# Attention, gated feed-forward and expert layer on one core: how the first unit is laid out, and who waits for the last scatters

## What is computed

```python
scores = scale * q @ k.T;  mask = (rel >= 0) & (rel < 64)      # rel = row - column
attn = softmax(where(mask, scores, -1e9)); a = attn @ v         # -> x [2304, 512]
xn = x / sqrt(mean(x*x) + 1e-6) * rms_g
y = (silu(xn @ w_gate) * (xn @ w_val)) @ w_out                  # 512 -> 1536 -> 512
e = argmax(y @ wg2);  p = softmax(y @ wg2)[e]
out[token] = p * (relu(y[token] @ w1[e]) @ w2[e])               # 512 -> 1024 -> 512
```

## Time and profile before

| | us |
|---|---|
| median of 3 runs | 842.87 (842.76 to 847.07) |
| the profiled execution | 843.32 |
| its span in the trace | 841.3 |

### The profile page before, as it was taken

The page is one execution under the profiler, slowest core; times in us unless marked ns, Lnnn a source line. Parts: engine busy times, 40 slices in busy tenths (PEclk is TensorE's granted clock), DMA queues, the critical chain, the costliest instruction groups (busy, mean ns, idle before and its releaser), DMA issues.

```text
span 841.3 us, 15268 instructions
## 1 busy us (share of the span) xinstructions
PE 818.7 (97%) x4803; PEld 732.0 (87%) x4804; DVE 483.2 (57%) x977; ACT 287.1 (34%) x664; POOL 214.3 (25%) x194
## 2 busy tenths in 40 slices
PE   6989999999999999999999999999999999999995
PEld 6877889999999999999999999998888888888884
DVE  5878822447764866676486667735315545564351
ACT  5767621321122121213212223334415435443440
POOL 5267799403000200300030000050831111111100
PEclk9999999999999999999999999999999999999998
DMA  6898880002002000200110012206354643654100
GB/s 207 252 316 260 300 328 39 1 1 76 1 0 76 1 1 3 76 1 1 34 42 1 1 39 101 100 28 239 118 180 150 217 156 138 248 192 178 53 19 20
DMA packets 38598, 88.22 MB, mean 105 GB/s; under 512 B 4030, under 2 KB 13246, under 8 KB 38016
## 3 DMA queue, kind: packets, MB, share of 16 engines
q1 hardware_dynamic: 33488, 72.89, 25.2%
q0 software_dynamic: 3360, 10.23, 3.4%
q10 hardware_dynamic: 1680, 4.21, 1.5%
HBM read 73.16 MB, written 14.94 MB: 105 GB/s over the span
## 4 chain that ended last, share of the span: by engine, by line
PE 92%; DMA 3%; ACT 1%; DVE 1%; issue 1%; POOL 1%; SPq 0%; POOLq 0%; ACTq 0%
PE ps L956 27%; PE ps L958 27%; PE ps L957 27%; PE ps L1094 2%; DMA kt<-kT 2%; PE ps L901 2%; PE ps L921 1%; PE ps L897 1%; PE ps L1015 1%; DMA xT_rows<-xo 1%; PE ps L909 1%; ACT pr L688 1%; PE ps L1131 0%; DVE nmax L1195 0%; PE ps L887 0%
## 5 line engine op out<-in xcount | busy, mean ns | idle before, releaser
L956 PE MATMUL ps<-xn_hi,GV_hi 128*128 128x384 f32 x576 | 195.6, 340 | 0.5 <-ACT pr L688 0.4
L958 PE MATMUL ps<-xn_hi,GV_lo 128*128 128x384 f32 x576 | 193.3, 336 | 0.0
L957 PE MATMUL ps<-xn_lo,GV_hi 128*128 128x384 f32 x576 | 193.0, 335 | 0.0
L956 PEld LDWEIGHTS ps<-xn_hi,GV_hi 128*128 128x128 f32 x576 | 108.2, 188 | 4.6 <-issue 0.6
L957 PEld LDWEIGHTS ps<-xn_lo,GV_hi 128*128 128x128 f32 x576 | 108.2, 188 | 3.3
L958 PEld LDWEIGHTS ps<-xn_hi,GV_lo 128*128 128x128 f32 x576 | 108.1, 188 | 0.0
L1291 DVE CUSTOM_DVE_ANT_0 ps<-ysb,wrb 128x512 f32<-128x512 f32 x120 | 91.9, 766 | 6.0 <-ACT ysb L750 1.0
L737 ACT ACTIVATE sig<-ps 128x384 f32<-128x384 f32 x72 | 35.4, 492 | 168.6 <-PE ps L958 168.5
L743 ACT ACTIVATE h_hi<-ps 128x384 fp32r<-128x384 f32 x72 | 35.4, 491 | 165.6 <-DVE ps L1261 165.6
L958 PE MATMUL ps<-Wo_hi,h_lo 128*128 128x512 f32 x216 | 85.5, 396 | 0.0
L957 PE MATMUL ps<-Wo_lo,h_hi 128*128 128x512 f32 x216 | 85.3, 395 | 0.0
(11 more groups left out here) (163 smaller groups left out, 1393.8 us busy)
## 6 DMA issues: line engine op xcount, KB each, us to landing
EW_raw<-w SPq DMA_DIRECT2D x32, 1024.0 KB, 5.7
vt<-vW SPq DMA_DIRECT2D x32, 192.0 KB, 5.1
qraw<-qT SPq DMA_DIRECT2D x16, 288.0 KB, 4.3
kt<-kT SPq DMA_DIRECT2D x16, 288.0 KB, 4.2
xT_rows<-xo SPq DMA_DIRECT2D x16, 288.0 KB, 3.6
y_rows<-ysb SPq DMA_DIRECT2D x6, 768.0 KB, 4.1
xraw<-xT_rows SPq DMA_DIRECT2D x5, 768.0 KB, 5.6
vt<-vW SPq DMA_DIRECT2D x16, 128.0 KB, 4.2
```

Source lines behind the costliest of these rows:

```text
L956: nc.tensor.matmul(out, a_hi, b_hi, start=start, stop=False)
L957: nc.tensor.matmul(out, a_hi, b_lo, start=False, stop=False)
L958: return nc.tensor.matmul(out, a_lo, b_hi, start=False, stop=stop)
```

## The change

At the head: q and k of unit 0 are loaded in two pieces each, the first job's columns (`FIRST`, three blocks, 192 columns) and the rest (`REST`, 384 columns). SP issues q's two pieces and k's rest before it raises its semaphores; ACT issues k's first piece before anything else, and `gvec` and `wr` only behind its first six jobs. `heads` is filled by VectorE with four fills; POOL cuts wider masks of 192 columns on all partitions in three selects, of which each half of the partitions takes its own 128 columns, and rounds the identity itself. VectorE copies the first mask, lays out the first piece of unit 0, copies the second mask, lays out the rest, and raises eight of its semaphores only then. TensorE multiplies job 0's scores before it adds the mask to them; in all other jobs the mask still comes first. POOL lays out unit 1 behind VectorE's lay-out, and waits for `gvec` and `wr` at unit 14.

In the middle: VectorE works out, for each of the four `osb` buffers, up to which count `o_out` must come (`landed_i`), and reads the four values into registers ahead of the slots.

At the tail: POOL waits for no landing. Its nested conditions are turned round, so that the last scatter stands in a condition of its own (`used == s + 1`) behind the block of the further levels. VectorE waits, behind its own last conditions, for the four counts and does a small instruction after each wait.

```diff
@@ build @@
-        mask_raw = r.take("mask_raw", 2, KEYS)
+        mask_raw = r.take("mask_raw", 2, WIN + KEYS)
@@ SP @@
+            sp.dma_start(qraw[0][:, FIRST], qT[0][:, FIRST]).then_inc(q_first, 16)
+            sp.dma_start(qraw[0][:, REST], qT[0][:, REST]).then_inc(q_in[0], 16)
+            sp.dma_start(kt[0][:, REST], kT[0][:, REST]).then_inc(k_in[0], 16)
             for s_ in (y_stored, *xT_out):
                 sp.sem_inc(s_, 16)
...
-            load_q(0, 0)
-            load_k(0, 0)
@@ POOL @@
-            for t, x in ((heads, 1.0), (ident, 0.0), (mask_raw, 0.0)):
-                g.memset(t[:], x).then_inc(blank, 1)
+            for t in (mask_raw, ident):
+                g.memset(t[:], 0.0).then_inc(blank, 1)
...
-            for half in halves:
...
+            select(mask_raw[:, 0, :], consts, compare_op=ALU.is_ge, fill=MASKED, base=0, pattern=[[-1, WIN + KEYS]],
+                   channel_multiplier=1)
+            select(mask_raw[:, 1, :], compare_op=ALU.is_gt, fill=MASKED, base=0, pattern=[[1, WIN + KEYS]],
+                   channel_multiplier=-1)
+            select(mask_raw[:, 1, :], consts, compare_op=ALU.is_ge, fill=MASKED, base=WIN, pattern=[[-1, WIN + KEYS]],
+                   channel_multiplier=1)
             select(ident[:], compare_op=ALU.not_equal, fill=1.0, base=0, pattern=[[-1, P]], channel_multiplier=1)
+            g.tensor_scalar(ident_r[:], ident[:], 1.0, 1.0, ALU.mult, ALU.mult).then_inc(mask_ready, 1)
...
-            lay_out_q(0)
+            pool.wait_ge(heads_set, 4)
+            pool.wait_ge(qbd_ready, done(2))
             lay_out_q(1)
...
-                with pool.If(used > s):
-                    if s + DEEP - 1 < SLOTS:
-                        with pool.If(used > s + DEEP - 1):
-                            gather(s + DEEP - 1)
+                if s + 1 < SLOTS:
+                    with pool.If(used > s + 1):
+                        if s + DEEP - 1 < SLOTS:
+                            with pool.If(used > s + DEEP - 1):
+                                gather(s + DEEP - 1)
+                        scatter(s)
+                        last_rows(s + 1)
+                with pool.If(used == s + 1):
                     scatter(s)
-                    if s + 1 < SLOTS:
-                        last_rows(s + 1)
-                    stored(s)
 
             last_rows(LEAST)
-            for s in range(LEAST - DEEP, LEAST):
-                stored(s)
@@ ACT @@
+            act.dma_start(kt[0][:, FIRST], kT[0][:, FIRST]).then_inc(k_first, 16)
@@ TensorE @@
-            pe.wait_ge(consts, 1)
-            pe.wait_ge(mask_ready, 3)
+            pe.wait_ge(qbd_first, 2)
+            pe.wait_ge(k_first, 16)
+            add_scores(0, 0, True)
+            pe.wait_ge(consts, 3)
+            pe.wait_ge(mask_ready, 5)
+            add_masks(0, False).then_inc(s_ready, 1)
             for j, u, b in jobs(0, 2 * JOBS):
-                scores(j, u, u, b, 16)
+                if j > 0:
+                    scores(j, u, u, b, 16, 1 - u)
@@ VectorE @@
+            for a, (half, _) in enumerate(of_half):
+                for b in range(2):
+                    nc.vector.memset(heads[half, b:b + 1], float(a == b)).then_inc(heads_set, 1)
+            for s_ in (max_ready, rden_ready, p_ready, pt_copied, rrms_ready, xn_step, xn_ready):
+                dve.sem_inc(s_, LEAD)
+            dve.wait_ge(consts, 1)
+            for half, cols in of_half:
+                nc.vector.tensor_copy(mask[half, 0, :], mask_raw[half, 0, cols]).then_inc(mask_ready, 1)
+            dve.wait_ge(heads_set, 4)
+            dve.wait_ge(q_first, 16)
+            lay_out_first(FIRST, qbd_first)
+            dve.wait_ge(consts, 2)
+            for half, cols in of_half:
+                nc.vector.tensor_copy(mask[half, 1:, :], mask_raw[half, 1:2, cols].to_broadcast([WIN, BPJ, KEYS])).then_inc(mask_ready, 1)
+            dve.wait_ge(q_in[0], 16)
+            lay_out_first(REST, qbd_ready)
+            for s_ in (silu_ready, h_ready, lo_ready, xsT_ready, h2T_ready, osb_ready, onehot_ready, logit_step):
                 dve.sem_inc(s_, LEAD)
...
+            link(v.tensor_tensor(landed[:], start[:, E:E + 1].to_broadcast([P, DEEP]), tile_no[:, 0:DEEP], ALU.subtract))
+            link(v.tensor_scalar(landed_i[:], landed[:], float(DEEP - 1), None, ALU.add))
+            link(v.tensor_scalar(landed_i[:], landed_i[:], -DEEP, None, ALU.bitwise_and))
...
             used = used_tiles(dve)
+            landings = [dve.value_load(landed_i[0:1, u:u + 1], min_val=LEAST // DEEP * DEEP, max_val=SLOTS + DEEP - 1)
+                        for u in range(DEEP)]
...
+            for u in range(DEEP):
+                dve.wait_ge(o_out[u], 16 // DEEP * landings[u])
+                v.tensor_scalar(closing[:, u:u + 1], landed[:, u:u + 1], 1.0, None, ALU.mult)
```

More of the change, by code:

```diff
@@ L96 @@
 STRIP_PAIRS = 3, 5, 7
+FIRST, REST = slice(0, BPJ * WIN), slice(BPJ * WIN, S)
 LAST_TAIL = NCH
@@ L236, in build @@
         start_i = rb.take("start_i", E + 1, dt=I32)
+        landed, landed_i = rb.take("landed", DEEP), rb.take("landed_i", DEEP, dt=I32)
+        closing = rb.take("closing", DEEP)
         ended, eid_f = rb.take("ended", SLOTS, E), rb.take("eid_f", SLOTS)
@@ L479, in _, with select @@
             g = nc.gpsimd
[L480 to L485, removed]
-            for t, x in ((heads, 1.0), (ident, 0.0), (mask_raw, 0.0)):
-                g.memset(t[:], x).then_inc(blank, 1)
+            def select(t, ready=None, **what):
+                ins = g.affine_select(out=t, in_=t, **what)
+                if ready is None:
+                    link(ins)
+                else:
+                    ins.then_inc(ready, 1)
@@ L495, in _ @@
-            halves = [slice(a * WIN, (a + 1) * WIN) for a in range(2)]
-            for half in halves:
[L498 to L505, removed]
+            select(mask_raw[:, 0, :], consts, compare_op=ALU.is_ge, fill=MASKED, base=0, pattern=[[-1, WIN + KEYS]],
+                   channel_multiplier=1)
@@ L716, in pair_of_units @@
                     copy_o(*job_before(j, i, O_LAG), 16 * pair + 16 if i >= O_LAG else 16 * pair)
+            act.dma_start(gvec[:], rms_g).then_inc(small_in, 16)
+            act.dma_start(wr[:], wg2.rearrange("(k p) e -> p k e", p=P)).then_inc(small_in, 16)
             with act.Fori(1, STRIP_PAIRS[0]) as pair:
@@ L887, in mean_squares, with add_masks, add_scores @@
                 nc.tensor.matmul(ps[:, MISC, 0:CH], ones_r[:].bitcast(F32), ssq[:], start=True, stop=True).then_inc(misc_ready, 1)
[L890 to L894, removed]
+            def add_masks(b, start):
                 masks = mask[:, min(b, 1):min(b, 1) + BPJ, :].rearrange("p i c -> p (i c)")
-                nc.tensor.matmul(ps[:, S_BANK + b, 0:BPJ * KEYS], ident_r[:], masks, start=True, stop=False)
+                return nc.tensor.matmul(ps[:, S_BANK + b, 0:BPJ * KEYS], ident_r[:], masks, start=start, stop=not start)
+            def add_scores(u, b, start):
                 for i in range(BPJ):
@@ L901, in scores @@
                     last = nc.tensor.matmul(ps[:, S_BANK + b, i * KEYS:(i + 1) * KEYS], qbd[u][:, k, :],
-                                            kt[u][:, k0:k0 + KEYS], start=False, stop=(i == BPJ - 1))
-                last.then_inc(s_ready, 1)
+                                            kt[u][:, k0:k0 + KEYS], start=(start and i == 0),
+                                            stop=(not start and i == BPJ - 1))
+                return last
+            def scores(j, n, u, b, loads, at=0):
+                if b == at:
+                    pe.wait_ge(qbd_ready, done(2 * n + 2))
+                    pe.wait_ge(k_in[u], loads)
+                pe.wait_ge(exp_ready, done(j - 2))
+                add_masks(b, True)
+                add_scores(u, b, False).then_inc(s_ready, 1)
             def weights_T(j, u, b):
@@ L1182, in _, with lay_out_first @@
         def _(dve):
-            for s_ in (max_ready, rden_ready, p_ready, pt_copied, rrms_ready, xn_step, xn_ready,
-                       silu_ready, h_ready, lo_ready, xsT_ready, h2T_ready, osb_ready, onehot_ready, logit_step):
+            def lay_out_first(cols, ready):
+                for a in range(2):
+                    nc.vector.tensor_scalar(qbd[0][:, cols.start // WIN:cols.stop // WIN, a * WIN:(a + 1) * WIN],
+                                            qraw[0][:, cols].rearrange("p (i r) -> p i r", r=WIN),
+                                            heads[:, a:a + 1], SCALE, ALU.mult, ALU.mult).then_inc(ready, 1)
+            of_half = [(slice(a * WIN, (a + 1) * WIN), slice(a * WIN, a * WIN + KEYS)) for a in range(2)]
+            for a, (half, _) in enumerate(of_half):
[15 more added lines that the diff above has]
+            for s_ in (silu_ready, h_ready, lo_ready, xsT_ready, h2T_ready, osb_ready, onehot_ready, logit_step):
                 dve.sem_inc(s_, LEAD)
```

15 lines of the change are left out of this document (4 added, 11 removed).

## The result

The kernel before took 844.97 us in this comparison (4 runs) and the changed one 855.65 (4 runs, 853.82 to 857.05): the ratio is **1.0131**, with a 95% interval of 1.0106 to 1.0156. It is slower by 11 us where 4.4 us faster was forecast, outside the range, and on the side that was given 2 in 100. The page of the changed kernel (its profiled execution took 853.82) begins like this: busy time by engine against the earlier trace rows, and from part 2 TensorE and its granted clock in 40 slices of 21.3 us.

A forecast was written before the change was run, and what follows sets the result against it. TensorE, busy for 97% of the span, was taken to bound the kernel. Head 2.0 us and tail 2.4 us, 4.4 together, off a median of 842.87 gave 838.5 us, with a range of 836.6 to 841.0.

The forecast's parts named there:

- the side that was given 2 in 100: Whole kernel: slower than before by over 0.5%, past 847.1 us, chance 0.02.
- part 2's first: Middle, near 590 us: three more linked VectorE instructions cost 0.2 us each, 0.6 in all.
- rival 4: Head: unit 1's k or q comes late, TensorE stops before job 3 and loses the clock: 844 us, chance 0.03.
- The cover: Middle: added VectorE work hides, as TensorE waits for nothing from 115 to 826 us and needs tile 2's low halves later.
- The four register loads: Middle, before the slots: four loads take 2.6 us, covered by 0.6, cost nil; uncovered, up to 2.6.
- Part 1: Head: loading unit 0 in pieces and scores before mask start job 1 2.0 us sooner, bounds 1.2 to 2.7.
- the other way of rival 3: Head: early scores don't help the clock rise, it comes no sooner than 10.5; head 1.1 less, 839.6 us.
- Part 3: Tail: POOL's DRAIN starts under the last scatter and still takes 3.51, ending at 838.7 instead of 841.1: 2.4 us won.
- Rivals 1 and 2: Tail: branch stalls or DRAIN counts from landing, 840.1 us (0.18); DRAIN ends as before, only head won, 840.9 (0.10).
- Rival 3: Clock: with the program 2 us earlier, the half-speed stretch costing 1.7 us may be missed: 836.8 us, chance 0.19.
- The prediction's sign of being wrong: Attention: the forecast is wrong if TensorE's sum of waits there grows; no size given.

The follow-up runs named there:

- e7: Changed kernel with the three added instructions behind the first `osb`; the first has two SBUF inputs, the others go through PSUM: 854.33 us, one run.
- e3: Changed kernel, the three added instructions at their place, but the value between second and third in PSUM: 840.58 us, ratio 0.996.
- e1: Changed kernel with the three added instructions moved up in front of GpSimd's gathers, behind the copy to `start_i`: 840.38 us, ratio 0.9952.
- e5: Kernel before with the new head alone, without the three added instructions and with the old tail: ratio 0.9957.
- e6: Kernel before with the new tail alone and the three added instructions placed early, behind `start_i`: ratio 0.9959.
- e11: Repeat of e6 (new tail alone on the kernel before), on one chip with e9: ratio 0.997.
- e2: Kernel before with only the three added instructions, at the change's place: 860.09 us, ratio 1.0177.
- e8: Changed kernel, GpSimd waiting behind its second subtraction until `landed_i` is there: 853.31 us, one run.
- e9: Repeat of e1 (changed kernel, three added instructions early): 839.78 us, ratio 0.9945.
- e4: Changed kernel, GpSimd waiting behind its first subtraction until `landed_i` is there: 846.56 us, ratio 1.0038.

## Why the prediction was wrong

**The step that failed** is part 2's first: "Three more linked instructions on VectorE near 590 us, 0.2 each, 0.6 in all". The first and the last took 0.15 and 0.17. The one between took 14.09, of which 13.4 reached TensorE and drew 3.1 more at the half clock. I took a price from the size of the work, and the cover from the waits of TensorE; I asked of GpSimd only what it waits for, not what VectorE shares with it. No bounds were drawn for this step at all. None of the five rivals contains the mechanism; rival 4, the one on the slower side, put the danger at the head. The kernel's description had the same gap: it lets the engines meet only at semaphores, and here GpSimd held VectorE without one. Both the danger and a small case of the hold stood in the trace of before, GpSimd's rows first, then VectorE's, then `gate_hi` by its tile:

```profile
587.02 0.95 POOL L611 DMA_INDIRECT xs<-y_rows,gidx  x1 [22.71 <-DVE gidx L1367]
...
590.92 13.72 POOL L626 TENSOR_TENSOR EW_lo<-EW_raw,EW_hi 128x2048 fp32r<-128x2048 f32 x3
...
587.59 0.37 DVE L1334 CAST gate_hi<-gate 128x3 fp32r<-128x3 f32 x1
...
L1334 DVE CAST gate_hi<-gate x2: 176/272/368, 543.4 to 587.6; 128x15 fp32r<-128x15 f32 x1, 128x3 fp32r<-128x3 f32 x1
```

The cast `gate_hi` takes 0.18 over 15 columns at 543.4, with GpSimd at rest, and 0.37 over 3 columns under a gather: it ends at 587.96, the gather at 587.97.

The Trainium skill states the mechanism in "SBUF — State Buffer", section Who interferes with whom: VectorE's second pair of ports belongs to GpSimd too and is locked exclusively; a tensor_scalar, copy or cast from SBUF to SBUF in a two-port mode takes it, and a VectorE instruction with two SBUF inputs contends with a GpSimd instruction that reads SBUF, while one SBUF input outside those modes does not. The traces agree in all three: 14.09 us (the addition), 13.61 (e7), and, with one SBUF input and the other in PSUM, 0.69 (`xsT_lo` in e3). Where the page says that who issues first has the pair "for the whole instruction", the measurement goes further: VectorE's instruction began at 586.98, before the first subtraction (587.61) and under a gather, and it was held over three instructions, not one. A reader who priced one subtraction would have said 4.5 us of wait, and the run says 13.4.

**The cover.** "Beside a TensorE that waits for nothing between 115 and 826" is true of the kernel before, and of e1 and e3 between 560 and 640. But behind the three instructions VectorE's queue holds `osb`, then `h2T_lo`, and TensorE has next to no slack there: of 14.09 us held, 0.7 were hidden. That TensorE needs the second tile's low halves "only behind the gate table's 18 matmuls" was right, but it looked past `osb`, and those matmuls cover less than a microsecond. The four register loads themselves did what was forecast: 0.30 each in e1, no wait of TensorE around them.

**Part 1** was right. 2.0 us was forecast, with bounds of 1.2 to 2.7; job 5's mask shows 2.3. The landing came at 3.1 (issued at 0.74, 2.4 to land), the lay-out ran 3.26 to 3.99 and the first score started at 4.05; forecast were 3.6, 4.15 for the end of the lay-out, and 4.4. Two terms were off and made up for each other: an instruction over 192 columns takes 0.37, not 0.25, and the landing came 0.5 sooner. Rival 4's condition did not arise (job 3 at 8.62, no wait for unit 1). The gain isn't the same in every trace: job 5's mask stands at 12.65 in e5 and 12.75 in e1, only 1.6 and 1.5 sooner than before, because a mask still takes 0.67 at 9.06 in e5, and 0.42 only from 10.81 on (in the changed kernel from 8.62, before from 10.97). There the full pace comes no sooner than before, as in the other way of rival 3.

**Part 3** was right in mechanism and size: 2.4 forecast, 2.4 in the rows of after, e1 and e6. Rivals 1 and 2 fell. The price weighed against the change (a stall at a branch, 840.1) was not paid: GpSimd's last branches stand at 846.9 to 847.0, in front of the scatter's start, and its DRAIN at 847.2. VectorE's 2.9 us between branch and DRAIN held 0.75 of `osb`. Whether its stall is still there can't be seen, because VectorE now waits for the landing until 849.7 anyway; its DRAIN starts at 850.1 and ends ahead of GpSimd's.

**Rival 3** was right that the fall of the clock moves, and right in its price; that a whole fall is saved, no trace shows. It is at 85 to 89 before, 83 to 87 after and in e3, 58 to 62 in e5. In e6 and e11 there is none in attention, but one comes at 573 to 577, at the same price of 1.7. e1, e2, e8 and e9 have one in attention and this one. TensorE had been busy without a break from 548 on (e1, e6, e8), and did half as many matmuls at the lower clock; first e8, then e4 for the same stretch:

```profile
574.00:576.00 2.00, 2.00 (x6) 1.57 (x5) 0.00 (x0) 0.00 (x0) 0.00 (x0) 0.50 1.03 402
...
574.00:576.00 2.00, 2.00 (x12) 1.63 (x11) 1.73 (x9) 1.30 (x1) 0.00 (x0) 1.00 1.05 397
```

The prediction's sign of being wrong, a grown sum of waits in attention, shows in part of the traces: the idle time is 5.1 in the changed kernel (before 5.9), but 7.4 in e1 and 7.1 in e9.

With the three instructions moved (e1, e9) the time is 4.1 to 4.6 us under before, around the forecast of 4.4 for everything but the step that failed. There is luck in how well it hits. In the profiled executions of e1 and e9 the head won 1.5 and 1.8 by job 5's mask, and idle time and the second half-clock stretch took 3 us back, so that their spans are only 1.0 and 1.6 under before's. And the forecast time itself, 838.5, was not reached (840.38 and 839.78): before, 842.87 in the three runs it was counted from, measured 844.4 to 845.1 in the later ones.

## What to carry to other kernels

An added VectorE instruction, however small, is priced by what GpSimd does at that moment. Look at GpSimd's timeline for a run of SBUF instructions without a gap, with an indirect gather ahead of it counted in. If there is one, keep one operand of the instruction in PSUM (one input and the output counted), or move it in front of the run and the gather. The price is the whole run of GpSimd's instructions, and whatever stands behind on VectorE's queue pays it. A stop of TensorE is then counted with the half-clock stretch behind it: the two together were 1.1 to 1.5 times the stop here (e2, e4).

## What was not expected of the hardware

- An elementwise instruction over 4 columns took 5.2, 9.6 and 14.1 us beside one, two and three GpSimd instructions of 4.5 us, and ended 0.04 us or less behind GpSimd's last. VectorE was not served between them.
- It began each time under GpSimd's indirect gather. At 0.17 us it would have been through at 587.15 in the changed kernel, 0.46 us ahead of the first subtraction: so the hold set in under the gather and went over to the subtractions. A gather alone held `gate_hi` in the trace of before (0.37 instead of 0.18).
- Not everything is held by a gather. `landed`, with two SBUF inputs, took 0.15 under one (586.79); `row_gate`, also with two, took 0.64 under one in the trace of before (588.76); and the cast `first`, started 0.06 behind a gather's start (586.70), took 0.18.
- The trace shows such a wait as busy time of VectorE: its 59% on the page hold 13.9 us in which it did nothing.
- After a stop of 13.4 us TensorE ran 6.1 us at 1.2 GHz in the changed kernel and 3.5 in e2, after 12.9 some 5.8 (e7), after 4.5 some 4.1 (594.8 to 598.9 in e4), after 8.9 some 4.1: the length behind the stop doesn't follow the stop.
- At 573 us the granted clock fell to 0.50 for some 3.5 us in six traces (e1, e2, e6, e8, e9, e11) with no wait of TensorE in front of it.
- GpSimd's closing DRAIN ended 3.5 us behind the end of the last scatter where it started under the scatter (847.2, 835.6 in e1, 836.7 in e6). With the wait for the landing between, it took 3.5 from its own start.
